# One unrolled program of 144 attention tiles in place of five stages, with a batch's mixing chain in one PSUM bank beside the last feed-forward steps of the batch ahead

## The reference

```python
scores = scale * np.matmul(q, k.transpose(0, 1, 3, 2))
kth = np.partition(scores, -top_k, axis=-1)[..., -top_k:-top_k + 1]
scores = np.where(scores >= kth, scores, -1000000000.0)
attn = np.exp(scores - np.max(scores, axis=-1, keepdims=True))
attn = attn / (np.sum(attn, axis=-1, keepdims=True) + 1e-09)
x = np.matmul(attn, v)                      # then (batch, 576, 512)
```

```python
gate = 1.0 / (1.0 + np.exp(-gate_pre))      # gate_pre: 5-tap convolution of x
x = gate * (x @ w_val) @ w_out
u = x + np.real(np.fft.fft(np.fft.fft(x, axis=1), axis=2))
un = (u - mean) / np.sqrt(var + 1e-06)
out = u + np.maximum(un @ w_ch1, 0.0) @ w_ch2
```

## Time and profile before

| quantity | value |
|---|---|
| median of 3 runs | 1224.27 us (1223.94 to 1225.94) |
| profiled execution's own time | 1226.49 us |
| its span, first to last instruction | 1224.7 us |
| mean granted TensorE clock | 0.938 |
| PE busy | 1055.4 us (86%) |
| DVE busy | 906.8 us (74%) |
| ACT busy | 604.9 us (49%) |
| POOL busy | 552.8 us (45%) |

### The profile page before, as it was taken

How to read it: one execution, slowest core, us unless ns; L and a number is a source line. 1 busy time by engine, 2 the same in 40 slices (tenths; PEclk the granted TensorE clock), 3 DMA queues, 4 the chain that set the end, 5 groups by cost and what they waited for, 6 DMA issues and landing times. The chain is left out here.

```text
span 1224.7 us, 20633 instructions
## 1 busy us (share of the span) xinstructions
PE 1055.4 (86%) x6864; PEld 864.3 (71%) x6864; DVE 906.8 (74%) x2008; ACT 604.9 (49%) x1253; POOL 552.8 (45%) x704
## 2 busy tenths in 40 slices
PE   2865556589989999799899999899899998998998
PEld 2554445477578888686588888786687887747897
DVE  6999999998899989397999987597999841020000
ACT  2676655455466655344566654444666541112221
POOL 2666655343566454243655453344655441133221
PEclk9887666789999999899999999999999999998999
DMA  8656363041167686330367674320575663306984
GB/s 245 187 171 187 129 198 98 25 152 36 30 229 224 218 270 208 94 106 29 100 222 239 251 228 156 135 74 10 176 240 201 226 212 107 114 1 237 331 310 140
DMA packets 81195, 200.46 MB, mean 164 GB/s; under 512 B 8384, under 2 KB 26560, under 8 KB 81088
## 3 DMA queue, kind: packets, MB, share of 16 engines
q1 hardware_dynamic: 81088, 199.11, 49.5%
HBM read 177.58 MB, written 21.50 MB: 163 GB/s over the span
## 5 line engine op out<-in xcount | busy, mean ns | idle before, releaser
L981 POOL TENSOR_TENSOR prob<-s_sb,prob 128x576 f32<-128x576 f32 x144 | 213.1, 1480 | 258.8 <-ACT prob L685 245.0
L824 DVE MAX8 top<-rest 128x8 f32<-128x576 f32 x432 | 304.8, 747 | 0.0
L818 DVE MATCH_REPLACE8 rest<-top,rest 128x576 f32<-128x576 f32 x288 | 211.7, 743 | 0.0
L617 PE MATMUL p_m<-w_st,hid_hi 128*128 128x512 f32 x640 | 201.2, 396 | 2.9 <-POOL hid_lo L1046 2.5
L606 PE MATMUL p_m<-un_hi,w_st 128*128 128x320 f32 (+1 forms) x1024 | 166.7, 305 | 21.1 <-ACT hid_hi L738 12.7
L1046 POOL TENSOR_TENSOR hid_lo<-hid,hid_hi 128x256 fp32r<-128x256 f32 (+1 forms) x128 | 104.9, 820 | 152.2 <-ACT hid_hi L738 151.5
L606 PEld LDWEIGHTS p_m<-un_hi,w_st 128*128 128x128 f32 x1024 | 143.5, 191 | 32.0 <-issue 19.6
L685 ACT ACTIVATE prob<-s_sb,bias 128x576 f32<-128x576 f32 x144 | 111.1, 772 | 101.2 <-POOL bias L977 99.7
L463 PE MATMUL p_s<-k_hi,q_st 128*128 128x512 f32 (+1 forms) x320 | 115.8, 364 | 47.7 <-ACT s_sb L675 13.2
L702 ACT ACTIVATE pT<-p_t 128x640 f32<-128x640 f32 x144 | 100.6, 699 | 107.8 <-PE p_t L478 106.4
L497 PE MATMUL p_t<-pT,v_sb 128*64 128x128 f32 (+1 forms) x1600 | 109.1, 289 | 50.5 <-ACT pT L702 36.8
(11 more groups left out here) (84 smaller groups left out, 1727.1 us busy)
## 6 DMA issues: line engine op xcount, KB each, us to landing
w_st<-w_split SPq DMA_DIRECT2D x256, 512.0 KB, 4.5
w_split<-w_st SPq DMA_DIRECT2D x32, 512.0 KB, 3.0
q_raw<-qT SPq DMA_DIRECT2D x64, 144.0 KB, 3.3
k_raw<-kT SPq DMA_DIRECT2D x64, 144.0 KB, 3.4
w_raw<-w_ch SPq DMA_DIRECT2D x32, 256.0 KB, 3.5
v_sb<-v SPq DMA_DIRECT2D x16, 256.0 KB, 3.9
wslot<-w_val SPq DMA_DIRECT2D x4, 1024.0 KB, 7.4
wslot<-w_out SPq DMA_DIRECT2D x4, 1024.0 KB, 5.4
```

The lines of the kernel that those rows point to most:

```text
L617: mm = pe.matmul(mbank(j), h[b][:, P * j:P * j + P], w2_st[(i - 1) % NB][:, w, :], start=f == 1 and part == 0, stop=f == FC and part == 2)
L818: dve.match_replace(rest[tt % 2][:, :], top[tt % 4][:, 8 * n - 8:8 * n], src[:, :], LOWEST).then_inc(s_chain, 1)
L824: found = dve.max(top[tt % 4][:, 8 * n:8 * n + 8], rest[tt % 2][:, :])
L981: pool.tensor_tensor(prob[t % 3][:, 0:S], s_sb[t % NS][:, :], prob[t % 3][:, 0:S], ALU.subtract).then_inc(s_arg, 1)
```

## The change

There are no stages any more: each engine runs one straight program over slots 0 to 150 and what follows, with one barrier at the end. The steps of batch b start in slot 36(b+1)+7, as before, but the last nine `ch1` steps (f = 8 to 16) of a batch are no longer in its own 36 slots: they stand between the chain steps of the next batch. For the last batch there is nothing to follow, so its steps run alone, one to a slot, with the nine steps of batch 2 between them.

To keep three sums alive beside a chain, the banks are dealt out anew. Hidden chunks have bank 2, sums have banks 0, 1 and 3 (three tiles in `ch0`, now 320 tokens wide; two in `ch1`, now 256), and the whole mixing chain has bank 3 alone. `val` is cut into two halves per chunk (257 and 319 tokens, in natural order; DVE's gating puts them into the folded order in one or two pieces) where it was four pieces (256, 256, 63 and 1 column). Every chain step on PE now waits for the copy of the chain step ahead of it. Convolution of the last chunk goes to slots 44 and 45 of a batch, the gate is made chunk by chunk, x_new is six rotating buffers, and w2_st has three buffers instead of four.

```diff
-STEPS = [("val", c) for c in range(KC)] + [("zed", m) for m in (2, 0, 1)]
-STEPS += [("seq", 0), ("proj", 0), ("proj", 1), ("seq", 1), ("proj", 2), ("proj", 3), ("seq", 2), ("trn", 0), ("proj", 4),
-          ("trn", 1), ("idle", 0)]
-for f in range(FC + 1):
-    STEPS += [("ch0", f)] + ([("trn", f // 3 + 1)] if f in (3, 6, 9) else [])
-STEPS += [("ch1", f) for f in range(FC + 1)]
-COST = {"idle": 3.0, "val": 3.9, "zed": 3.4, "seq": 2.6, "proj": 3.4, "trn": 0.6, "ch0": 3.1, "ch1": 3.5}
-SEQ_BANK = [3, 2, 1]
-PROJ_BANK = [0, 1, 3, 0, 2]
+GROUPS = [[0, 2, 4], [1, 3]]
+SUM_BANK = [0, 1, 3]
+HIDDEN_BANK = 2
+CHAIN_BANK = 3
+CHAIN = [("val", j) for j in range(2 * KC)] + [("zed", m) for m in (2, 0, 1)]
+CHAIN += [("seq", 0), ("proj", 0), ("proj", 1), ("seq", 1), ("trn", 0), ("proj", 2), ("proj", 3), ("seq", 2), ("trn", 1),
+          ("proj", 4), ("trn", 2)]
+FILL_AFTER = [None, ("val", 3), ("val", 7), ("zed", 1), ("seq", 0), ("proj", 1), ("proj", 3), ("proj", 4), ("trn", 2)]
+LAG = len(FILL_AFTER)
+COST = {"val": 2.2, "zed": 3.5, "seq": 2.6, "proj": 3.5, "trn": 0.6, "ch0": 3.9, "ch1": 2.8}
+def batch_steps(b):
+    late = [("ch1", b - 1, f) for f in range(FC + 1 - LAG, FC + 1)] if b else []
+    out = []
+    for where in [None] + CHAIN:
+        if where is not None:
+            out.append((where[0], b, where[1]))
+        if where in FILL_AFTER and late:
+            out.append(late.pop(0))
+    out += late
+    out += [("ch0", b, f) for f in range(FC)] + [("trn", b, 3), ("ch0", b, FC), ("trn", b, 4)]
+    out += [("ch1", b, f) for f in range(FC + 1 - (LAG if b < B - 1 else 0))]
+    return out
...
                     def values(c):
-                        if c >= 2:
-                            pe.wait_ge(m_gv, c - 1)
-                        at, x0 = (c % 2) * 2 * BANK, TAPS - 1
-                        for o0, o1, src in ((0, HALF, slice(x0 + 1, x0 + 1 + HALF)),
-                                            (HALF, 2 * HALF, slice(x0 + S - 1, x0 + S - 1 - HALF, -1)),
-                                            (2 * HALF, S - 1, slice(x0 + HALF + 1, x0 + S - HALF)),
-                                            (S - 1, S, slice(x0, x0 + 1))):
-                            mm = chain(p_m, P, at + o0, at + o1, lhs, [x_new[:, k, src] for k in range(KC)])
+                def values(b, j):
+                    if j:
+                        pe.wait_ge(m_gv, upto_gv(b, j))
+                    n0, n1 = VAL[half]
+                    mm = chain(mbank(CHAIN_BANK), P, 0, n1 - n0, [wslot[:, k, P * c:P * c + P] for k in range(KC)],
+                               [x_new[(PAIRS * b + k) % NX][:, TAPS - 1 + n0:TAPS - 1 + n1] for k in range(KC)])
...
+                def transpose_un(b, n):
+                    r = LN[n]
+                    pe.wait_ge(m_un, NR * b + r + 1)
...
+                def hidden(b, g, f):
+                    if f == 0:
+                        pe.wait_ge(m_unlo, NR * b + (NR if g else len(GROUPS[0])))
...
-            numbers = sorted(x.num for x in sems)
-            nc.gpsimd.sem_clear(range(numbers[0], numbers[-1] + 1))
-            nc.all_engine_barrier()
-        stage(0, None)
-        with nc.Fori(1, B - 1) as b:
-            stage(b, b - 1)
-        stage(B - 1, B - 2, ahead=False)
-        stage(None, B - 1)
```

More of the change, by code:

```diff
@@ new lines, in steps_by_slot @@
+def steps_by_slot():
+    out = {s: [] for s in range(ALL_TILES + ATTEND)}
+    for b in range(B):
+        steps = batch_steps(b)
+        start = NT * (b + 1) + ATTEND
+        if b == B - 1:
+            for n, step in enumerate(steps):
+                out[start + n] = [step]
+            break
+        total = sum(COST[x[0]] for x in steps)
+        spent, n = 0.0, 0
+        for i in range(NT):
+            while n < len(steps) and spent + COST[steps[n][0]] / 2 <= total * (i + 1) / NT:
+                out[start + i].append(steps[n])
+                spent += COST[steps[n][0]]
+                n += 1
+        out[start + NT - 1] += steps[n:]
@@ L163, in build @@
         pm = sb("pm", [P, 2, NCOS])
-        un = [sb(f"un{i}", [P, DM]) for i in range(2)]
+        un = [sb(f"un{i}", [P, DM]) for i in range(4)]
         stats = sb("stats", [P, NR, 6])
@@ new lines, in unit_due, with split_due, part_due, conv_due @@
+        def unit_due(s):
+            return due(s, ATTEND) and unit_end(s - ATTEND) is not None
+        def split_due(s):
+            p, i = divmod(s + 1, TILES)
+            return p if i == 0 and p < ALL_PAIRS else None
+        def part_due(s):
+            return s - SPLIT_AT if 0 <= s - SPLIT_AT < 2 * FC else None
+        def conv_due(s):
+            return [(b, c, taps) for b in range(B) for c, taps in CONV_AT.get(s - NT * b, [])]
+        def tanh_due(s):
+            return [(b, TANH_AT[s - NT * b]) for b in range(B) if s - NT * b in TANH_AT]
@@ L939, in _ @@
-                    if first:
-                        split_low(0)
-                    for s in plan:
-                        if mlp and s == ATTEND:
-                            conv(-1, range(TAPS))
-                        if due(s, RECIP):
-                            reciprocal(s - RECIP)
-                        if due(s, SELECT) and (s - SELECT) % 2:
-                            select(s - SELECT, 0)
-                        if due(s, SELECT + 1) and (s - SELECT - 1) % 2:
-                            select(s - SELECT - 1, 1)
-                        if split_due(s) is not None:
-                            split_low(split_due(s))
-                        for what, n in plan[s]:
-                            step(what, n)
-                        for c, taps in CONV_AT.get(s, []) if att else []:
-                            conv(c, taps)
@@ new lines, in _ @@
+                for part in hid_hi + hid_lo:
+                    dve.memset(part[:, WIDTH[0]:].bitcast(F32), 0.0).then_inc(s_zero, 1)
+                dve.memset(factors[:, 0:1], -SCALE).then_inc(s_zero, 1)
+                dve.memset(factors[:, 1:2], BIG).then_inc(s_zero, 1)
+                dve.memset(power[:, :], -0.5).then_inc(s_zero, 1)
+                split_low(0)
+                for s in plan:
+                    if due(s, RECIP):
+                        reciprocal(s - RECIP)
+                    if due(s, SELECT) and (s - SELECT) % 2:
+                        select(s - SELECT, 0)
+                    if due(s, SELECT + 1) and (s - SELECT - 1) % 2:
+                        select(s - SELECT - 1, 1)
+                    if split_due(s) is not None:
+                        split_low(split_due(s))
+                    for x in plan[s]:
+                        step(*x)
+                    for b, c, taps in conv_due(s):
+                        conv(b, c, taps)
@@ L1094, in tables @@
+        numbers = sorted(x.num for x in sems)
+        assert numbers == list(range(numbers[0], numbers[-1] + 1))
+        nc.gpsimd.sem_clear(range(numbers[0], numbers[-1] + 1))
+        nc.all_engine_barrier()
 def tables():
```

1363 lines of the change are left out of this document (654 added, 709 removed).

## The result

The changed kernel takes 1277.69 us (median of 4 runs, 1273.98 to 1280.26) against 1224.11 for the kernel before (4 runs, 1220.58 to 1225.94): 1.0439 times as long, 95% interval 1.0403 to 1.0475. The forecast was 1231 with a range up to 1246. The profiled execution took 1280.26 us, its span is 1278.5.

The account below looks back on a forecast made before the run. PE was taken to bound the kernel from 251 us on, DVE before that and in changed batch 0. 249.5 + 250 + 261 + 253 + 217.7 = 1231.2, 6.5 above 1224.7: median 1231, own range 1227 to 1238, 8 in 10 1206 to 1246.

Parts of the forecast that it names:

- First slots: First stage, bound by DVE: its last slot, starting at 245.17, is short and ends at 249.5 us.
- `val`: Cut of `val` on PE: halves of 1.81 and 2.24 us, a chunk 4.05 instead of 5.40, 5.4 us less a batch.
- Tail: Batch 3's steps running alone: 193.6 of PE work, 18.4 of waits, 4.7 at the end, 1 of clock: 217.7 us.
- Six waits behind a half: Tail, chain steps directly behind a `val` half: 0.7 us each, 4.2; the longer second convolution slot adds 1.2.
- the low clock: Tail: 7 us of loss already in the last stage's 175.6 us of PE work, and 1 more.
- slots 80 to 83: Batch 1, seven `val` halves: DVE takes 37 us, PE has 27 to 28 of work, which leaves 9 idle.
- 19 us of idle in all: Batch 1 on PE: 9 in the `val` slots, 3 before `ch1` 0, 2 in pairs, 5 elsewhere; 242 + 19 = 261.
- the three pairs: Batch 0, slots 43, 44 and 46 with two halves: DVE waits 2.25 us for each second half, 6.9 together.
- slot 51: Batch 0, two projections in one slot: DVE waits for PE, 6.9 us together.
- The clock rival: Clock falls in the chain; nine second halves each 2 us longer, two thirds on the path, 12: 1243 us. Chance 0.15.
- The faster rival: Chain waits are hidden as PE and DVE slide: 1197.5 us at the far end, 1214 with half hidden. Chance 0.33.
- Costed at nothing: Three `w2_st` buffers: loads, needed 6.9 us later, land in 5.2 to 5.9; extra instruction loads of unrolled code also cost nothing.

Follow-up runs that it names:

- e4_warm: Changed kernel plus three fp32 constant products on PE, read by nobody, behind every `val` half of batch 0: 1274.6 us against 1277.7.
- e9_two_lag2: Changed kernel with two alternating banks for the chain and two late `ch1` steps (behind `proj` 4 and `trn` 2) instead of nine: 1222.0 us.
- e10_two_lag2_trn: e9_two_lag2 with transposes 3 and 4 ahead of `ch0` steps 6 and 11 instead of at the end of `ch0`: 1213.1 us, 0.9901 times the kernel before.

## Why the prediction was wrong

**First slots, right.** DVE's slot 43 begins at 247.8 (249.5 forecast), and the first scores of the pair slots have no idle time ahead of them. The stage's end wait of the earlier trace rows is gone as the forecast said.

**`val`, right.** Halves of 1.90 to 2.00 and 2.41 us, printed with their drain, against 1.81 and 2.24. With the drain a chunk is 4.4, so where its halves stand apart the cut saves 1.0 of the 5.40 and not 1.35.

**Tail, right in its waits.** Six waits behind a half, forecast at 4.2 and 1.2, are 4.3; those behind zed and proj, forecast at 0.8 and 1.0 each, are 0.7 and 0.95:

```profile
1068.26 2.41 PE L479 MATMUL p_m<-x_new,wslot 128*128 128x319 f32 x8 [0.51 <-DVE gv L862]
1071.31 2.00 PE L479 MATMUL p_m<-x_new,wslot 128*128 128x257 f32 x8 [0.64 <-DVE gv L862]
1074.77 2.42 PE L479 MATMUL p_m<-x_new,wslot 128*128 128x319 f32 x8 [1.46 <-DVE gv L862]
...
1097.32 3.72 PE L479 MATMUL p_m<-wfeat,gate 128*128 128x257 f32 x16 [0.68 <-ACT z L691]
...
1118.83 3.70 PE L479 MATMUL p_m<-wslot,gv 128*128 128x512 f32 x8 [0.95 <-DVE u_one L829]
```

All idle time there is 17.1 us (18.4 forecast). PE's busy time is 190.7 where 194.6 was forecast: I had charged 8 us for the low clock, but half clock was granted for 8.3 us of the tail (17.5 before), with PE at work in 5.9 of them, which is 3 us. So most of the 5 us by which the tail came out shorter is a term of the clock that was too large there, while the batches had none. The second bank took 13.2 us off the tail; the Trainium skill's rule of reading another bank than the one written (page "PSUM — Partial Sum Buffer", section "Summary: rules for kernel authors") had been worked out at 12 there, and the run agrees.

**The failed step: PE's and DVE's work in the batches was taken at its old speed, with each wait charged once and to one engine.** In batch 1 I laid out slots 80 to 83 and found 9 us of PE idle; the row (516 to 566) says 11.0:

```profile
PE p_m L479 <- DVE gv L862: 11.0, 3, 5.3
```

I charged PE 19 us of idle in all; it is 25. But I then added PE's 242 us of work unchanged, and it became 250; in batch 2 it is 248.6 instead of 236.6, in batch 0 234.8 instead of 218. Batches 0, 1 and 2 have 31, 17 and 21 us more at half clock than before, and PE was at work in 29, 13 and 17 of them; half of that is 14, 7 and 9, most of the growth of 17, 8 and 12. In batches 1 and 2 the growth is 20 of the 34 us of the miss, of which the clock is some 15, and 14 are idle time.

In batch 0, where DVE bounds, I charged the three pairs 6.9 us and slot 51 6.9; they are 12.7 and 9.7. The half clock makes 5.6 of it (e4_warm). The batch's other waits of DVE are 17 instead of 10.5, and its busy time is 231.7 instead of 225.2, of which some 3 belong to the first slots. That late steps lengthen batches 1 and 2, which give as much work as they get, I had costed at nothing: two banks with and without late steps show 2.7 and 7.8 us there.

**The rivals.** The clock rival had the mechanism: granted clock under 0.9 in slots 43 to 47 and 80 to 83, and it was 0.83 from 245 to 305 us and 0.89 from 518 to 565. Its price for a second half was right too (2 us forecast, 1.9 measured). It counted nine halves, 12 us, and left out that attention, late steps and the first half behind each wait run slow as well: 60 us more at half clock, 50 of them with PE at work, are 25 us of PE time. The Trainium skill's section on a clock that swings with idle time between matmul groups (page "TensorE: Matmul & The Clock Gate", section "A second HAM failure mode: psum-queue depth-cycling") spoke for this rival; the runs agree with it beyond what I gave it, and in this kernel the swing is as large with alternating banks (92.6 us) as with one (92.2). The faster rival, waits that slide under each other, has nothing for it: PE is idle 25 us in batch 1, and it needed less than 10. The chance of 0.15 for the clock was set from the loop's stages of before, where PE hardly stood; the change itself made the stretches in which it stands.

**The range.** The forecast's own range of 1227 to 1238 doesn't follow from the ends as it says: taken one at a time they give 1219 to 1239.

**Costed at nothing, right.** With three `w2_st` buffers no DMA appears as a releaser of the sums (their only wait is 0.2 us for POOL in the tail).

## What to carry to other kernels

When a buffer is made single, write down for each slot what both engines wait for: a copy that stands behind a long unrelated job of its engine makes the two take turns, and the remedy is a second buffer or the copy's place in that job's order, not both. If PE then stands in a slot, price a lower clock for all its work around there and not just for the instruction that waited: here the clock in such slots was 0.83 to 0.90 on the mean, and it took as much from batches 1 and 2 as the added idle time. The same idle time in shorter pieces can cost less: the early transposes left it as it was and gave 9 us. Work that is moved to fill waits should go only where a wait was measured: nine steps lost 10 us with two banks, two steps beside the one long wait won 5 by the ratios.

## What the runs showed of the hardware

I had not expected how far idle time inside slots reaches: in the pair slots PE was granted 0.83 and 0.90 of its clock, where a chain without such waits had 0.99, and 5 us of standing cost another 2 in the half behind it. Behind an idle time of 5.28 us a half took 4.35 us instead of 2.41, behind 0.5 to 1.5 us in the tail it stayed at 2.41. The length of the one idle time does not decide it: in batch 0 a half behind 2.09 us took 4.00, and the next one, behind 1.71, 2.42. Products that nobody reads bring the clock back (0.97 from 245 to 305 us in e4_warm), but with 22 us of them in the way the kernel gained 3 us, which is not clear of the noise. The runs of a kernel spread differently, 11 us over 11 runs of e9_two_lag2 and 4.5 us over 5 of e10_two_lag2_trn; that the clock makes the difference is not shown.
